# In the first MLP ScalarE casts the up weights' high parts, and the third token pair's first sums stand amid the second pair's chain

## The chip, the cores and the metric

The kernel runs on one core of a Trainium2 chip. The metric is the device time of one execution in microseconds; the median of three runs is given. Engines: TensorE (PE, matmuls; PEld, its weight loads), VectorE (DVE), ScalarE (ACT), GpSimd (POOL) and SyncE (SP, which issues most transfers). Each engine runs its own program in order; semaphores join them.

## What is computed

Clustered attention, then two MLPs, on 2 x 768 tokens of width 512, all in float32:

```python
h = x @ w_in                              # first MLP, d_ff 2048
g = h * (1.0 / (1.0 + np.exp(-1.702 * h)))
x = g @ w_out
...
h = x @ w_in                              # second MLP, d_ff 1024
e = np.exp(h - np.max(h, axis=-1, keepdims=True))
solu = h * (e / (np.sum(e, axis=-1, keepdims=True) + 1e-09))
mu = np.mean(solu, axis=-1, keepdims=True)
var = np.mean((solu - mu) ** 2, axis=-1, keepdims=True)
out = ((solu - mu) / np.sqrt(var + 1e-06) * g_ln) @ w_out
```

The attention (16 heads, keys of a query's own cluster only) is not touched by the change, except that its last turn also prepares the first weights of the first MLP.

## The kernel before

Each operand of a matmul is split in a high part (a cast to fp32r) and a low part (the exact value less the high one); a product is three matmuls: high x high, low x high, high x low. The cast and the subtraction are instructions of their own.

**First MLP.** There are three blocks (`bl`) of 512 tokens. A unit is one hidden tile of 128 columns; each block has 16, in pairs `m` (or `at`) with `u` = 0 and 1, so 48 units in all (n = 2 `at` + `u`). TensorE does, in turn, `up` of one unit (12 matmuls, L578 to L580) and `down` of the unit two before (12 matmuls, L593 to L595). For each unit:
- SP loads 512 KB of up and down weights into one of four slots of `gelu_raw`, as soon as `downl` of the unit four before is done (L453).
- GpSimd, `split_up`: a tiny `wait_scrap` instruction (L1354) that carries the waits, the cast `uph` (L1401), the difference `upl` (L1403). Then `split_down` of the unit before: `wait_scrap`, `downh` (L1411), `downl` (L1413). `uph[u]` may be written when `up` of the unit two before is done, `downh[u]` when its `down` is.
- ScalarE, `gelu`: the Tanh into `gate` (L786), then, when VectorE has multiplied the gate (L1028), the cast `gh` (L790). VectorE then makes `gl` (L1031).

`gate` is one buffer; `uph`, `upl`, `gh` and `gl` have two each. Beside this VectorE and ScalarE prepare the second MLP's weights: VectorE in the first block (`split_down_rows`), both in the second (`rhs_high` on ScalarE, `rhs_low_part` and `rhs_sum` on VectorE). At the end of a block ScalarE copies the four accumulators (`x2_high`, L796). ScalarE's and GpSimd's programs for this stage are partly loops.

**Second MLP.** There are six pairs of token tiles (`it` 0 to 5, tiles `u` 0 and 1). The up projection of a pair is a Strassen-like scheme of 7 products, in the order ONE, SIX, FIVE, SEVEN, TWO, FOUR, THREE (L685 to L687), which share few PSUM banks: TWO of a pair waits until ScalarE has copied ONE (`one_copy`, L897), FOUR until VectorE has used SIX (`u2_sum`, L1221), THREE until it has used SEVEN (`u3_sum`, L1233; between them `u4_sum`, L1228). Then come `c11`, `c21`, `c22`, `c12` (L1237 to L1251), and for each tile: max (L1260), exp (ACT, L904), solu and its mean (L1266 to L1274), the sum of squares (ACT, L919), variance (L1288, L1291), the root (POOL, L1508), the norm (L1296 to L1300, whose last instruction goes over the whole tile), transposes (PE, L705), `lnt_high` (ACT, L912) and `lnt_low` (DVE, L1280), and the down projection (L716 to L718), which `copy_out` (L927, L929) stores. GpSimd splits the next pair's left operands (L1495 to L1504), in its order before the two roots of the pair. TensorE does the transposes and the down projections of the pair before behind a pair's products. The order on each engine is written out by hand.

Of the kernel before, what the change touches and what calls it, by code (L numbers as in the profile page):

```python
# [16 lines left out]
def clustered_attention_two_mlps(nc, q_t, k_t, v_r, cent, w_gelu, w_ln, gains, out):  # L17
# [11 lines left out]
    DM = H * D  # L29
# [20 lines left out]
    with ExitStack() as ctx:  # L50
# [174 lines left out]
        uph_done = sem("uph_done")  # L225
# [27 lines left out]
        stat_step = sem("stat_step")  # L253
# [213 lines left out]
        def _(pe):  # L467
# [101 lines left out]
            def up(bl, m, u):  # L569
                n = bl * FF + m * 2 + u  # L570
                pe.wait_ge(uph_done, n + 1)
                pe.wait_ge(upl_done, n + 1)

                pe.wait_ge(gate_done[u], FREE + bl * (FF // 2) + m)
                tok = bass.ds(bl * BL, BL)
                for k in range(KT):
                    cols = slice(k * P, (k + 1) * P)
                    nc.tensor.matmul(hidden[u], uph[u][:, cols], xh[:, k, tok], start=k == 0, stop=False)  # L578
                    nc.tensor.matmul(hidden[u], uph[u][:, cols], xl[:, k, tok], start=False, stop=False)  # L579
                    last = nc.tensor.matmul(hidden[u], upl[u][:, cols], xh[:, k, tok], start=False, stop=k == KT - 1)  # L580
                last.then_inc(up_done[u], 1)
# [160 lines left out]
        def _(act):  # L742
# [38 lines left out]

            def gelu(at, u):
# [3 lines left out]
                nc.scalar.activation(gate[:], hidden[u], ACT.Tanh, scale=SLOPE / 2).then_inc(tanh_done, 1)  # L786
                act.wait_ge(gate_done[u], FREE + at + 1)
# [73 lines left out]
            with act.Fori(1, PER) as m:  # L861
                for u in range(2):
                    gelu(m, u)
            x2_high(0)
            for u in range(2):
                gelu(PER, u)
            act.wait_ge(ln_loaded, ITS * 16)
            for m in range(1, PER + 1):
                if m == PER:
                    x2_high(1)  # L870
                for u in range(2):
                    gelu(PER + m, u)
                    k, part = divmod((m - 1) * 2 + u, RHS_SLOTS)
                    if k < HK and part == 0:
                        rhs_high(B11, k, raw_unit(k, 0))
                    if k < HK and part == 1:
                        rhs_high(B21, k, raw_unit(HK + k, 0))
                    if k < HK and part == 2:
                        rhs_high(B22, k, raw_unit(HK + k, 1))
                    if k < HK and part == 4:  # L880
# [3 lines left out]
                    if k < HK and part == 5:  # L884
# [3 lines left out]
            with act.Fori(1, PER) as m:  # L888
                for u in range(2):
                    gelu((NBL - 1) * PER + m, u)  # L890
# [48 lines left out]
            for it in range(1, PAIRS):  # L939
                if it > 1:  # L940
                    one_copy(it)
                    lnt_high(it - 1, 0)
                for u in range(2):
                    exp_tile(it, u)
                    square(it, u)
                if it > 1:
                    copy_out(it - 2, 1)
                    lnt_high(it - 1, 1)
                copy_out(it - 1, 0)
                if it == 1:  # L950
                    lnt_high(0, 1)
# [8 lines left out]
        def _(dve):  # L960
# [241 lines left out]
            def solu_step(it, u):  # L1202
                return it * 8 + u * 3 + 2

            def variance_step(it, u):
                if it in (0, PAIRS - 1) and u == 1:
                    return it * 8 + 7
                return it * 8 + (6 if u else 3)

            def norm_step(it, u):  # L1210
                if it in (0, PAIRS - 1) and u == 0:
                    return it * 8 + 6
                return it * 8 + 6 + u + 1

# [48 lines left out]
            def solu_tile(it, u):  # L1263
# [8 lines left out]
                nc.vector.tensor_scalar(st(u, 5), st(u, 1), 1e-9, None, ALU.add).then_inc(stat_step, 1)  # L1272
                dve.wait_ge(stat_step, solu_step(it, u) - 1)
                nc.vector.reciprocal(st(u, 6), st(u, 5)).then_inc(stat_step, 1)  # L1274
# [9 lines left out]
            def variance(it, u):  # L1284
                dve.wait_ge(square_done, it * 2 + u + 1)
                dve.wait_ge(stat_step, solu_step(it, u))

                nc.vector.tensor_scalar(st(u, 7), st(u, 4), st(u, 6), st(u, 6), ALU.mult, ALU.mult  # L1288
                                        ).then_inc(stat_step, 1)
                dve.wait_ge(stat_step, variance_step(it, u))  # L1290
                nc.vector.tensor_scalar(st(u, 8), st(u, 7), 1.0 / F2, 1e-6, ALU.mult, ALU.add).then_inc(var_done, 1)  # L1291

            def norm_tile(it, u):
                t = it * 2 + u
                dve.wait_ge(root_done, t + 1)
                nc.vector.reciprocal(st(u, 10), st(u, 9)).then_inc(stat_step, 1)  # L1296
                dve.wait_ge(stat_step, norm_step(it, u))
# [37 lines left out]
        def _(pool):  # L1335
# [228 lines left out]
```

## Time and profile before

| | us |
|---|---|
| median of 3 runs | 671.42 (671.18 to 672.23) |
| the profiled execution | 671.9 |
| its span, first to last instruction | 670.1 |
| TensorE matmuls busy | 634.8 (95%) |
| weight loads busy | 532.0 (79%) |
| GpSimd busy | 492.6 (74%) |
| VectorE busy | 471.5 (70%) |
| ScalarE busy | 331.8 (50%) |
| first MLP | about 260 to 540 |
| second MLP | from about 525 on |

Records of matmuls overlap, since they are pipelined: in the first MLP one takes 0.39 us and the next starts 0.23 later, so a busy share near 100% says little there. The weight loads, one for each matmul, show TensorE's pace. The granted clock was 1.00 of full speed from 100 us on.

### The profile page before, as it was taken

What the parts mean: (1) busy time and instruction counts of PE and PEld (TensorE: products, weight loads), DVE (VectorE), ACT (ScalarE), POOL (GpSimd) and SP (SyncE); (2) the same over time, 40 slices, a digit from 0 to 9 for tenths busy, and PEclk for the clock granted to TensorE, in tenths of its full rate; (3) what the DMA queues carried; (4) which work ended last, traced back from release to release, by engine and by line L of the source; (5) the groups of instructions that cost most, each with busy time, mean ns of one, the idle gap of its engine ahead of it and who ended that gap; (6) DMA issues with size and microseconds to landing.
All of it is one profiled execution on the core that took longest, in us unless ns stands there. A gap on an engine that the chain in (4) does not pass through costs nothing.

```text
span 670.1 us, 11363 instructions
## 1 busy us (share of the span) xinstructions
PE 634.8 (95%) x3245; PEld 532.0 (79%) x3245; DVE 471.5 (70%) x805; ACT 331.8 (50%) x661; POOL 492.6 (74%) x680
## 2 busy tenths in 40 slices
PE   5679999999999999999999999999999997999998
PEld 1369989898989888788878778788888886888876
DVE  3769999999999985666646655734555587777660
ACT  1269999989999984222223322332222244443241
POOL 2667798797887977888878898988888778477100
PEclk9779999999999999999999999999999999999999
DMA  8866544545545421122232222222220000000001
GB/s 283 254 182 145 149 132 109 146 107 141 133 109 149 113 110 63 65 98 96 105 109 68 97 86 94 94 94 95 94 94 31 1 0 17 32 17 17 31 33 47
DMA packets 26937, 64.31 MB, mean 96 GB/s; under 512 B 3873, under 2 KB 10017, under 8 KB 26913
## 3 DMA queue, kind: packets, MB, share of 16 engines
q1 hardware_dynamic: 24896, 60.09, 30.1%
q10 hardware_dynamic: 2016, 3.93, 1.6%
q8 instruction: 11, 0.18, 0.1%
q14 instruction: 14, 0.11, 0.0%
HBM read 46.60 MB, written 4.72 MB: 77 GB/s over the span
## 4 chain that ended last, share of the span: by engine, by line
PE 66%; ACT 11%; DVE 8%; issue 8%; DMA 3%; POOL 3%; DVEq 1%; ACTq 0%; SPq 0%; POOLq 0%
PE banks L563 7%; PE banks L578 6%; PE banks L580 6%; PE banks L593 6%; PE banks L579 6%; PE banks L595 6%; PE banks L594 6%; PE banks L548 4%; ACT probs L805 4%; ACT probs_th L816 3%; PE banks L718 3%; PE banks L717 3%; PE banks L716 3%; PE banks L685 2%; PE banks L687 2%
## 5 line engine op out<-in xcount | busy, mean ns | idle before, releaser
L1057 DVE TENSOR_TENSOR probs_tl<-banks,probs_th 128x384 fp32r<-128x384 f32 x192 | 100.5, 546 | 11.3 <-ACT probs_th L816 8.8
L1037 DVE TENSOR_REDUCE neg_max<-banks 128x1 f32<-128x768 f32 x96 | 91.0, 949 | 10.2 <-PE banks L535 8.3
L816 ACT CAST probs_th<-banks 128x384 fp32r<-128x384 f32 x192 | 83.1, 486 | 23.3 <-PE banks L548 22.1
L1354 POOL TENSOR_TENSOR wait_scrap<-half_power 128x1 f32<-128x1 f32 x176 | 47.6, 270 | 63.8 <-DVE row_inv L1051 31.6
L1031 DVE TENSOR_TENSOR gl<-gate,gh 128x512 fp32r<-128x512 f32 x48 | 41.8, 871 | 71.4 <-ACT gh L790 71.4
L805 ACT ACTIVATE probs<-banks,neg_max 128x768 f32<-128x768 f32 x96 | 88.1, 918 | 6.1 <-DVE neg_max L1037 6.1
L1430 POOL TENSOR_SCALAR probs<-probs,row_inv 128x768 f32<-128x768 f32 x96 | 87.1, 908 | 0.0
L548 PE MATMUL banks<-ident,probs 128*128 128x128 f32 x576 | 79.4, 274 | 0.6 <-ACT hot_t L759 0.6
L563 PE MATMUL banks<-probs_th,v_parts 128*128 128x384 f32 x192 | 70.5, 367 | 9.9 <-DVE x_sums L1064 9.9
L790 ACT CAST gh<-gate 128x512 fp32r<-128x512 f32 x48 | 29.8, 621 | 100.9 <-PE banks L595 62.6
L578 PE MATMUL banks<-xh,uph 128*128 (+1 forms) x192 | 76.6, 399 | 1.2 <-POOL upl L1403 1.2
L1413 POOL TENSOR_TENSOR downl<-gelu_raw,downh 128x512 fp32r<-128x512 f32 x48 | 74.2, 1547 | 4.0
L593 PE MATMUL banks<-gh,downh 128*128 128x512 f32 x192 | 76.0, 396 | 0.2
L580 PE MATMUL banks<-xh,upl 128*128 (+1 forms) x192 | 75.5, 393 | 0.0
L595 PE MATMUL banks<-gh,downl 128*128 128x512 f32 x192 | 75.4, 393 | 0.0
L579 PE MATMUL banks<-xl,uph 128*128 (+1 forms) x192 | 75.1, 391 | 0.0
L594 PE MATMUL banks<-gl,downh 128*128 128x512 f32 x192 | 75.0, 391 | 0.0
L548 PEld LDWEIGHTS banks<-ident,probs 128*128 128x128 f32 x576 | 69.2, 141 | 4.7 <-ACT hot_t L759 0.9
L1403 POOL TENSOR_TENSOR upl<-gelu_raw,uph 128x512 fp32r<-128x512 f32 x48 | 63.9, 1332 | 4.0
L786 ACT ACTIVATE gate<-banks 128x512 f32<-128x512 f32 x48 | 28.7, 598 | 76.6 <-PE banks L580 63.4
L563 PE MATMUL banks<-probs_tl,v_parts 128*128 128x384 f32 x192 | 65.3, 340 | 0.0
L531 PE MATMUL banks<-k_high,q_parts 128*128 128x384 f32 x192 | 56.5, 376 | 5.0 <-DMA k_low<-mask_rows 2.3
(144 smaller groups left out, 1415.0 us busy)
## 6 DMA issues: line engine op xcount, KB each, us to landing
gelu_raw<-w_gelu SPq DMA_DIRECT2D x48, 512.0 KB, 3.3
ln_raw<-w_ln SPq DMA_DIRECT2D x8, 512.0 KB, 4.5
pair_t<-q_t SPq DMA_DIRECT2D x4, 768.0 KB, 7.4
pair_t<-k_t SPq DMA_DIRECT2D x4, 768.0 KB, 8.2
kq_raw<-k_t SPq DMA_DIRECT2D x16, 192.0 KB, 3.5
kq_raw<-q_t SPq DMA_DIRECT2D x16, 192.0 KB, 3.7
q_parts<-k_high SPq DMA_DIRECT2D x16, 192.0 KB, 2.6
q_high<-k_high SPq DMA_DIRECT2D x16, 192.0 KB, 3.0
```

The costliest lines, as they stand in the source:

```text
L548: last = nc.tensor.transpose(pt_bank(n, c)[:, t * P:(t + 1) * P], probs[:, n % NP, k * P:(k + 1) * P], ident[:])
L563: last = nc.tensor.matmul(head_out, v_parts[j][:, i // 2].rearrange("p two d -> p (two d)"), part[half % 2][:, i // 2, :], start=i == 0, s ...
L578: nc.tensor.matmul(hidden[u], uph[u][:, cols], xh[:, k, tok], start=k == 0, stop=False)
L579: nc.tensor.matmul(hidden[u], uph[u][:, cols], xl[:, k, tok], start=False, stop=False)
L580: last = nc.tensor.matmul(hidden[u], upl[u][:, cols], xh[:, k, tok], start=False, stop=k == KT - 1)
L593: nc.tensor.matmul(acc[d], downh[u][:, cols], gh[u][:], start=first, stop=False)
L594: nc.tensor.matmul(acc[d], downh[u][:, cols], gl[u][:], start=False, stop=False)
L595: last = nc.tensor.matmul(acc[d], downl[u][:, cols], gh[u][:], start=False, stop=end)
L805: nc.scalar.activation(probs[:, n % NP, :].rearrange("p (c t) -> p c t", c=2), scores[n % 2], ACT.Exp, bias=neg_max[:, n % NP:n % NP + 1], ...
L816: nc.scalar.copy(probs_th[half % 2][:, c * CH:(c + 1) * CH, i * P:(i + 1) * P], pt_bank(n, c).rearrange("p (t s) -> p t s", t=CH)).then_in ...
L1037: nc.vector.tensor_reduce(out=neg_max[:, col], in_=scores[n % 2], op=ALU.max, axis=mybir.AxisListType.XY, negate=True).then_inc(max_done, 1)
L1057: nc.vector.tensor_tensor(probs_tl[half % 2][at], pt_bank(n, c).rearrange("p (t s) -> p t s", t=CH), probs_th[half % 2][at].bitcast(F32), ...
```

## The change

1. For units 4 to 47 the cast `uph` moves from GpSimd to ScalarE (`up_high`), directly behind the Tanh of the unit two before, with the wait for the load. GpSimd keeps the four casts of units 0 to 3, without their `wait_scrap`. `uph_done` becomes two semaphores.
2. ScalarE's loops over the first MLP are written out.
3. In the second MLP pair 2's `one_copy`, `u2_sum`, `u4_sum` and `u3_sum` are done amid pair 1's exp and solu, as is `lnt_high(0, 1)` and `lnt_low(0, 1)`; `norm_tile(1, 0)` comes behind `u3_sum(2)`.
4. The counting semaphore `stat_step` becomes four, one for each kind of small step.

```diff
             def up(bl, m, u):
                 n = bl * FF + m * 2 + u
-                pe.wait_ge(uph_done, n + 1)
+                pe.wait_ge(uph_done[u], bl * (FF // 2) + m + 1)
                 pe.wait_ge(upl_done, n + 1)
...
+            def up_high(at, u):
+                n = at * 2 + u
+                act.wait_ge(gelu_loaded[n % RAW], (n // RAW + 1) * 16)
+                nc.scalar.copy(uph[u][:], gelu_raw[:, n % RAW, 0:DM]).then_inc(uph_done[u], 1)
+
             def gelu(at, u):
                 act.wait_ge(up_done[u], at + 1)
 
                 act.wait_ge(gl_done, FREE + at * 2 + u)
                 nc.scalar.activation(gate[:], hidden[u], ACT.Tanh, scale=SLOPE / 2).then_inc(tanh_done, 1)
+                if at >= 1 and (at + 1) * 2 + u < NBL * FF:
+                    up_high(at + 1, u)
                 act.wait_ge(gate_done[u], FREE + at + 1)
...
             for it in range(1, PAIRS):
-                if it > 1:
-                    one_copy(it)
+                if it == 1:
+                    exp_tile(1, 0)
+                    lnt_high(0, 1)
+                    square(1, 0)
+                    one_copy(2)
+                    exp_tile(1, 1)
+                    square(1, 1)
+                    copy_out(0, 0)
+                else:
+                    if it > 2:
+                        one_copy(it)
                     lnt_high(it - 1, 0)
...
             for it in range(PAIRS):
-                u2_sum(it)
-                if it >= 2:
+                if it != 2:
+                    u2_sum(it)
+                if it >= 3:
                     norm_tile(it - 1, 0)
-                u4_sum(it)
-                u3_sum(it)
+                if it != 2:
+                    u4_sum(it)
+                    u3_sum(it)
                 if it == 1:
                     lnt_low(0, 0)
+                if it == 2:
+                    norm_tile(1, 0)
                 if it >= 1:
                     norm_tile(it - 1, 1)
...
                 variance(it, 0)
+                if it == 1:
+                    lnt_low(0, 1)
+                    u2_sum(2)
+                    u4_sum(2)
                 solu_tile(it, 1)
+                if it == 1:
+                    u3_sum(2)
                 if it in (0, PAIRS - 1):
                     norm_tile(it, 0)
                 variance(it, 1)
-                if it >= 1:
+                if it > 1:
                     lnt_low(it - 1, 1)
...
             def split_up(it, r):
                 u = r % 2
-                pool.wait_ge(gelu_loaded[r], (it + 1) * 16)
-                if exists(it, r, 2, RAW):
-
-                    pool.wait_ge(up_done[u], it * (RAW // 2) + r // 2)
-                carry_waits(STEPS + r)
                 raw = gelu_raw[:, r, 0:DM]
-                nc.gpsimd.tensor_scalar(uph[u][:], raw, 1.0, 1.0, ALU.mult, ALU.mult).then_inc(uph_done, 1)
-                pool.wait_ge(uph_done, it * RAW + r + 1)
+                if isinstance(it, int):
+                    pool.wait_ge(gelu_loaded[r], 16)
+                    if r >= 2:
+
+                        pool.wait_ge(up_done[u], r // 2)
+                    nc.gpsimd.tensor_scalar(uph[u][:], raw, 1.0, 1.0, ALU.mult, ALU.mult).then_inc(uph_done[u], 1)
+                pool.wait_ge(uph_done[u], it * 2 + r // 2 + 1)
                 nc.gpsimd.tensor_tensor(upl[u][:], raw, uph[u][:].bitcast(F32), ALU.subtract).then_inc(upl_done, 1)
```

GpSimd's loop over the first MLP, one unit, before (L1402, L1408 and L1412 only set up registers and waits):

```order
L1354 TENSOR_TENSOR wait_scrap<-half_power 128x1
L1401 TENSOR_SCALAR uph<-gelu_raw 128x512
L1402 ISA
L1403 TENSOR_TENSOR upl<-gelu_raw,uph 128x512
L1408 ISA
L1354 TENSOR_TENSOR wait_scrap<-half_power 128x1
L1411 TENSOR_SCALAR downh<-gelu_raw 128x512
L1412 ISA
L1413 TENSOR_TENSOR downl<-gelu_raw,downh 128x512
```

and now:

```order
L1408 TENSOR_TENSOR upl<-gelu_raw,uph 128x512
L1413 ISA
L1359 TENSOR_TENSOR wait_scrap<-half_power 128x1
L1416 TENSOR_SCALAR downh<-gelu_raw 128x512
L1417 ISA
L1418 TENSOR_TENSOR downl<-gelu_raw,downh 128x512
```

The first `wait_scrap` and the cast have left GpSimd's program; the rest keeps its order. On ScalarE the cast stands between the Tanh and `gh`, here at the start of the second block, now:

```order
L806 ACTIVATE x_sums<-banks 128x512 x4
L794 ACTIVATE gate<-banks 128x512
L788 CAST uph<-gelu_raw 128x512
L800 CAST gh<-gate 128x512
L794 ACTIVATE gate<-banks 128x512
L788 CAST uph<-gelu_raw 128x512
L800 CAST gh<-gate 128x512
```

VectorE from the max of tile (1,1) to the norm of (1,0), before (L1266 to L1274 solu, L1288 and L1291 variance, L1280 `lnt_low(0, 1)`, L1221, L1228 and L1233 the sums of pair 2, L1296 to L1300 the norm):

```order
L1260 TENSOR_REDUCE stat<-gelu_raw 128x1
L1288 TENSOR_SCALAR stat<-stat 128x1
L1291 TENSOR_SCALAR stat<-stat 128x1
L1266 ISA gelu_raw,stat<-gelu_raw,exp 128x1024
...
L1288 TENSOR_SCALAR stat<-stat 128x1
L1291 TENSOR_SCALAR stat<-stat 128x1
L1280 TENSOR_TENSOR xh<-banks,xh 128x1024
L1221 TENSOR_TENSOR hid<-banks,hid 128x512
L1296 RECIPROCAL stat<-stat 128x1
L1298 TENSOR_TENSOR stat<-stat 128x1
L1300 TENSOR_SCALAR gelu_raw<-gelu_raw,stat 128x1024
L1228 TENSOR_TENSOR hid<-banks,hid 128x512
L1233 TENSOR_TENSOR hid<-banks,hid 128x512
```

and now (L1275 `lnt_low`, L1216, L1223 and L1228 the sums, L1261 to L1269 solu, L1283 and L1286 variance, L1291 to L1295 the norm):

```order
L1255 TENSOR_REDUCE stat<-gelu_raw 128x1
L1283 TENSOR_SCALAR stat<-stat 128x1
L1286 TENSOR_SCALAR stat<-stat 128x1
L1275 TENSOR_TENSOR xh<-banks,xh 128x1024
L1216 TENSOR_TENSOR hid<-banks,hid 128x512
L1223 TENSOR_TENSOR hid<-banks,hid 128x512
L1261 ISA gelu_raw,stat<-gelu_raw,exp 128x1024
...
L1228 TENSOR_TENSOR hid<-banks,hid 128x512
L1283 TENSOR_SCALAR stat<-stat 128x1
L1286 TENSOR_SCALAR stat<-stat 128x1
L1291 RECIPROCAL stat<-stat 128x1
L1293 TENSOR_TENSOR stat<-stat 128x1
```

The low parts and two sums have moved ahead of the solu of (1,1), the third sum behind it. ScalarE at the same place, before (L904 exp, L919 square, L927 and L929 `copy_out(0, 0)`, L912 `lnt_high(0, 1)`, L897 `one_copy(2)`):

```order
L904 ACTIVATE exp,stat<-gelu_raw,stat 128x1024
L919 ACTIVATE gelu_raw,stat<-gelu_raw,stat 128x1024
L904 ACTIVATE exp,stat<-gelu_raw,stat 128x1024
L919 ACTIVATE gelu_raw,stat<-gelu_raw,stat 128x1024
L927 COPY gelu_raw<-banks 128x512
L929 DMA out<-gelu_raw 128x512
L912 CAST xh<-banks 128x1024
L897 COPY hid<-banks 128x512
```

and now:

```order
L906 ACTIVATE exp,stat<-gelu_raw,stat 128x1024
L914 CAST xh<-banks 128x1024
L921 ACTIVATE gelu_raw,stat<-gelu_raw,stat 128x1024
L899 COPY hid<-banks 128x512
L906 ACTIVATE exp,stat<-gelu_raw,stat 128x1024
L921 ACTIVATE gelu_raw,stat<-gelu_raw,stat 128x1024
L929 COPY gelu_raw<-banks 128x512
L931 DMA out<-gelu_raw 128x512
```

The two copies that stood last come in between the exp and the squares.

## Rows read from the trace of the kernel before

**Rows 1.** Stretches: us, busy time (x instructions) of PE, PEld, DVE, ACT, POOL, clock, DMA

```profile
275.41:330.49 55.08, 55.07 (x240) 45.02 (x240) 36.67 (x36) 12.19 (x20) 46.29 (x60) 1.00 0.28 95
353.15:435.78 82.63, 81.75 (x349) 64.79 (x349) 52.10 (x55) 25.58 (x44) 73.62 (x88) 1.00 0.26 89
443.91:510.30 66.39, 66.39 (x289) 54.16 (x288) 35.41 (x42) 15.23 (x25) 55.28 (x72) 1.00 0.26 87
```

**Rows 2.** Waits of PEld, 340 to 446 us: total us, times, longest

```profile
PEld banks L578 <- issue: 3.6, 8, 0.7
PEld banks L593 <- DVE gl L1031: 0.5, 1, 0.5
```

**Rows 3.** Timeline, first block's start: start us, us, engine, what [idle before]

```profile
272.77 0.38 POOL L1354 TENSOR_TENSOR wait_scrap<-half_power 128x1 f32<-128x1 f32 x1
...
275.41 0.19 PEld L578 LDWEIGHTS banks<-xh,uph 128*128 128x128 f32 x1 [0.87 <-issue]
```

**Rows 4.** Timeline of PEld, pair 2 of the second MLP

```profile
561.32 0.19 PEld L685 LDWEIGHTS banks<-rhs_h,lhs_h 128*128 128x128 f32 x1 [2.60 <-POOL lhs_l L1497]
561.42 0.19 PEld L686 LDWEIGHTS banks<-rhs_l,lhs_h 128*128 128x128 f32 x1
...
565.78 0.19 PEld L685 LDWEIGHTS banks<-rhs_h,lhs_h 128*128 128x128 f32 x1 [1.85 <-POOL lhs_l L1497]
...
567.04 1.03 PEld L705 LDWEIGHTS banks<-ident,gelu_raw 128*128 128x128 f32 x8
```

**Rows 5.** Timeline of ACT, pairs 1 and 2

```profile
557.56 1.15 ACT L919 ACTIVATE gelu_raw<-gelu_raw,stat 128x1024 f32<-128x1024 f32 x1 [1.49 <-DVE stat L1270]
...
559.70 1.01 ACT L912 CAST xh<-banks 128x1024 fp32r<-128x1024 f32 x1 [0.43 <-ACT gelu_raw L927]
560.61 0.59 ACT L897 COPY hid<-banks 128x512 f32<-128x512 f32 x1
```

**Rows 6.** Timeline of DVE, pairs 1 and 2

```profile
556.11 1.23 DVE L1266 CUSTOM_DVE_ANT_0 gelu_raw<-gelu_raw,exp 128x1024 f32<-128x1024 f32 x1 [0.93 <-ACT exp L904]
...
560.75 1.22 DVE L1280 TENSOR_TENSOR xh<-banks,xh 128x1024 fp32r<-128x1024 f32 x1 [1.45 <-ACT xh L912]
...
564.97 0.69 DVE L1233 TENSOR_TENSOR hid<-banks,hid 128x512 f32<-128x512 f32 x1
```

**Rows 7.** POOL's groups by form, 300 to 500 us: busy us, mean ns | idle

```profile
L1401 POOL TENSOR_SCALAR uph<-gelu_raw 128x512 fp32r<-128x512 f32 x36 | 25.3, 704 | 0.0
L1354 POOL TENSOR_TENSOR wait_scrap<-half_power 128x1 f32<-128x1 f32 x72 | 25.1, 348 | 23.5 <-PE banks L595 20.4 <-PE banks L580 2.9
```

**Rows 8.** ACT's groups by form, 300 to 500 us

```profile
L859 ACT CAST rhs_h<-ln_raw 128x512 fp32r<-128x512 f32 x14 | 8.2, 616 | 0.0
```

**Rows 9.** Timeline, start of the third block

```profile
441.58 0.60 ACT L786 ACTIVATE gate<-banks 128x512 f32<-128x512 f32 x1 [0.64 <-PE banks L580]
...
442.21 0.69 DVE L1028 SCALAR_TENSOR_TENSOR gate<-gate,banks 128x512 f32<-128x512 f32 x1 [5.52 <-ACT gate L786]
...
442.55 1.29 POOL L1403 TENSOR_TENSOR upl<-gelu_raw,uph 128x512 fp32r<-128x512 f32 x1
...
443.91 0.19 PEld L578 LDWEIGHTS banks<-xh,uph 128*128 128x128 f32 x1
```

**Rows 10.** Timeline, one unit of the second block

```profile
387.78 1.66 POOL L1413 TENSOR_TENSOR downl<-gelu_raw,downh 128x512 fp32r<-128x512 f32 x1
...
395.74 0.60 ACT L786 ACTIVATE gate<-banks 128x512 f32<-128x512 f32 x1 [2.13 <-PE banks L580]
```

**Rows 11.** The page's DMA issues: KB each, median us to landing

```profile
gelu_raw<-w_gelu SPq DMA_DIRECT2D x48, 512.0 KB, 3.3
```

**Rows 12.** Timeline of PE, transposes of tile (0,1)

```profile
552.60 1.03 PE L705 MATMUL banks<-ident,hid 128*128 128x128 f32 x8
```

**Rows 13.** Tile `gelu_raw`: ns min/median/max, first and last start

```profile
L1300 DVE TENSOR_SCALAR gelu_raw<-gelu_raw,stat x6: 810/814/1315, 563.0 to 648.4; 128x1024 f32<-128x1024 f32 x6
```

**Rows 14.** Timeline of DVE, low part of tile (1,0)

```profile
571.20 1.22 DVE L1280 TENSOR_TENSOR xh<-banks,xh 128x1024 fp32r<-128x1024 f32 x1
```

More of the change, by code:

```diff
@@ L224, in clustered_attention_two_mlps @@
         gelu_loaded = [sem(f"gelu_loaded{r}") for r in range(RAW)]
-        uph_done = sem("uph_done")
+        uph_done = two_sems("uph_done")
         upl_done = sem("upl_done")
@@ L252, in clustered_attention_two_mlps @@
         square_done = sem("square_done")
-        stat_step = sem("stat_step")
+        sum2_guarded = sem("sum2_guarded")
+        sum2_inverted = sem("sum2_inverted")
+        spread_scaled = sem("spread_scaled")
+        root_inverted = sem("root_inverted")
         var_done = sem("var_done")
@@ L859, in rhs_high @@
                 nc.scalar.copy(rhs_h[:, i, k, :], src).then_inc(rhs_high_done, 1)
-            with act.Fori(1, PER) as m:
-                for u in range(2):
[L863 to L874, printed above, removed]
+            for at in range(1, NBL * PER):
+                if at == PER + 1:
+                    act.wait_ge(ln_loaded, ITS * 16)
+                if at % PER == 0:
+                    x2_high(at // PER - 1)
+                for u in range(2):
+                    gelu(at, u)
+                    k, part = divmod((at - PER - 1) * 2 + u, RHS_SLOTS)
+                    if 0 <= k < HK and part == 0:
                         rhs_high(B11, k, raw_unit(k, 0))
-                    if k < HK and part == 1:
+                    if 0 <= k < HK and part == 1:
                         rhs_high(B21, k, raw_unit(HK + k, 0))
-                    if k < HK and part == 2:
+                    if 0 <= k < HK and part == 2:
                         rhs_high(B22, k, raw_unit(HK + k, 1))
-                    if k < HK and part == 4:
+                    if 0 <= k < HK and part == 4:
                         act.wait_ge(rhs_summed, k * 4 + 2)
@@ L883, in _ @@
                         rhs_high(T3, k, raw_unit(k, 1))
-                    if k < HK and part == 5:
+                    if 0 <= k < HK and part == 5:
                         act.wait_ge(rhs_summed, k * 4 + 4)
@@ L887, in _ @@
                         rhs_high(T4, k, raw_unit(HK + k, 0))
-            with act.Fori(1, PER) as m:
-                for u in range(2):
-                    gelu((NBL - 1) * PER + m, u)
             def one_copy(it):
@@ L939, in _ @@
             for it in range(1, PAIRS):
-                if it > 1:
-                    one_copy(it)
+                if it == 1:
[9 more added lines that the diff above has]
+                        one_copy(it)
                     lnt_high(it - 1, 0)
[L943 to L946, printed above, removed]
+                    for u in range(2):
+                        exp_tile(it, u)
+                        square(it, u)
                     copy_out(it - 2, 1)
                     lnt_high(it - 1, 1)
-                copy_out(it - 1, 0)
-                if it == 1:
-                    lnt_high(0, 1)
+                    copy_out(it - 1, 0)
             lnt_high(PAIRS - 1, 0)
@@ L1199, in st @@
                 return stat[:, u, i:i + 1]
[L1202 to L1213, printed above, removed]
             def quarter(it, u, c):
@@ L1270, in solu_tile @@
                 nc.vector.tensor_scalar(st(u, 3), st(u, 2), -1.0 / F2, None, ALU.mult).then_inc(mean_done, 1)
-                nc.vector.tensor_scalar(st(u, 5), st(u, 1), 1e-9, None, ALU.add).then_inc(stat_step, 1)
-                dve.wait_ge(stat_step, solu_step(it, u) - 1)
-                nc.vector.reciprocal(st(u, 6), st(u, 5)).then_inc(stat_step, 1)
+                nc.vector.tensor_scalar(st(u, 5), st(u, 1), 1e-9, None, ALU.add).then_inc(sum2_guarded, 1)
+                dve.wait_ge(sum2_guarded, t + 1)
+                nc.vector.reciprocal(st(u, 6), st(u, 5)).then_inc(sum2_inverted, 1)
             def lnt_low(it, u):
@@ L1295, in norm_tile @@
                 dve.wait_ge(root_done, t + 1)
-                nc.vector.reciprocal(st(u, 10), st(u, 9)).then_inc(stat_step, 1)
-                dve.wait_ge(stat_step, norm_step(it, u))
+                nc.vector.reciprocal(st(u, 10), st(u, 9)).then_inc(root_inverted, 1)
+                dve.wait_ge(root_inverted, t + 1)
                 nc.vector.tensor_tensor(st(u, 11), st(u, 10), st(u, 6), ALU.mult).then_inc(scale_done, 1)
```

6 lines of the change are left out of this document (3 added, 3 removed).

## The prediction

> **What bounds the kernel now.** I read the stretches first, then the waits of TensorE's weight loads, then the chain around the stalls. In the first MLP TensorE is nearly always busy, so what counts is how far it is from its own pace. One weight load belongs to each matmul, so the loads are a clock. The last block's stretch is the undisturbed pace: 66.39 us for 288 loads, 0.2305 us each, 5.53 us for the 24 matmuls of one hidden tile of 128 (a unit) [rows 1]. (The count in each row includes the load that starts at the window's end.) The second block's stretch took 82.63 us for 348 loads; at the last block's pace it would take 80.2, so it **lost 2.4 us**. The first block's stretch, 55.08 for 240 loads, lost nothing (55.3 at that pace). The list of waits says where: before the up matmuls (L578) 8 waits, 3.6 us, between 340 and 446 us, with "issue" as the cause, and one of 0.5 before L593 that is put down to VectorE's `gl` [rows 2]. "Issue" isn't a proof of GpSimd, but what an up matmul waits for is `upl`, GpSimd's last product of a unit.
>
> At the start of the first block the same wait is larger: the load at 275.41 came after 0.87 us of idling, right behind the `wait_scrap` of 0.38 us that began on GpSimd at 272.77, the cast and `upl` [rows 3].
>
> In the second MLP TensorE stands still twice, in the third token pair (pair 2): 2.60 us before the load at 561.32 and 1.85 before that at 565.78 [rows 4]. The engine named there (GpSimd) is a false lead: the first wait ends with ScalarE's copy `hid` (L897), which starts at 560.61 and takes 0.59 [rows 5]; the second with VectorE's third sum (L1233), 564.97 plus 0.69 [rows 6]. A wait shows 0.04 us more than it costs, since undisturbed loads lie 0.23 apart and last 0.19; and the load after a wait follows after 0.10 instead of 0.23. So the two cost 2.60 + 1.85 - 2 x 0.17 = **4.1 us**.
>
> **The change part by part: first MLP.** For 44 of 48 units GpSimd loses the cast `uph`, 704 ns in the mean between 300 and 500 us, and one `wait_scrap` of 348 ns [rows 7]: 1.05 us of the unit's 5.53. GpSimd's order is downl of one unit, then upl of the next, and the down part waits for TensorE to free `downh`; that loop is what came out longer than TensorE's pace when VectorE's extra work in the second block slowed GpSimd. With 1.05 us less in it, each of the eight waits (3.6/8, below 0.5 on average) goes. Value: 2.4 us. The wait at 275.41 goes too: `uph` for this unit can be cast after the Tanh of unit 2, before GpSimd is free at 272.77, and 1.0 us, the scrap's 0.38 [rows 3] and a cast of some 0.62 [rows 8], disappears. Value: 0.83 (its 0.87 less 0.04); but the first block then runs at 0.2305 a load, not 55.08/240, which gives back 0.24. From below the value of these three is nothing (if GpSimd isn't the cause), from above 3.3 with the smaller irregularities between the blocks.
>
> What ScalarE gets is 44 casts. The row for such a cast is 616 ns (`rhs_h`, same shape) [rows 8]. It stands between the Tanh (0.60) and `gh`, while VectorE multiplies the gate: undisturbed, `gh` starts some 1.35 us after the Tanh's start, after a Tanh of 0.60 and a gate of 0.69 [rows 9], and Tanh plus cast is over after 1.2. So it is hidden by VectorE's work. If that cover were gone, it would cost `gh` 0.6 us, which has to be ready for a down product over one unit later, so still nothing.
>
> Two places have no slack: the first units of blocks two and three. Their `uph` waits for the up product before last and is wanted one product later. Before, GpSimd began on it 0.1 us after the Tanh's start. Now it is Tanh, cast, `upl`: 441.58 + 0.55 + 0.62 + 0.05 + 1.29 = 444.1, and TensorE, which loaded at 443.91 [rows 9], loads at 444.2. I put +0.3 on this place, +0.1 on the one before (a wait there already), and the 0.5 before L593 stays, since VectorE's order is the same. First MLP: 2.4 + 0.8 - 0.24 - 0.4 = **2.5 us gained**.
>
> The cast also waits for its weights. The load into a slot goes out when `downl` of four units earlier ends (387.78 + 1.66 = 389.44) and lands after 3.3 us in the median, about 392.9; the Tanh behind which the cast stands is at 395.74 [rows 10, 11]. 3 us of slack: nothing. Queued behind a late one would be `gh`, then `gl`, then the down product.
>
> **Second MLP.** I follow the new order with the old durations. The transposes of tile (0,1) end at 553.63 [rows 12]. ScalarE copies them (L912) from 553.67, next instruction 0.91 later, as from 559.70 to 560.61 [rows 5]: the square of (1,0) starts at 554.58 and is done 1.25 later (1.15 [rows 5] and 0.1 for reading out its sum), 555.83; the copy of product ONE is done at 556.3 instead of 561.2; exp of (1,1) at 557.5. VectorE: variance to 556.3, `lnt_low` 1.2 [rows 6] to 557.5, first sum (0.69 as the third [rows 6], and the handover) to 558.2, second to 558.95, then solu of (1,1), whose mean is there 1.4 us later (1.23 and the small operations), 560.4, third sum to 561.3. The square of (1,1) lies beside it, 560.4 to 561.7; variance to 562.15; norm of (1,0): 0.4 of small operations and a tile that takes between 0.81 and 1.31 [rows 13]; I take 1.31, since GpSimd takes up its splits at just that time: 563.9.
> TensorE goes from 558.76 (561.32 less the wait) through TWO and FOUR without a wait, is at THREE at 561.5 (third sum 561.3) and at the transposes of (1,0) at 562.9. They wait for the norm: load at 564.0 instead of 567.04 [rows 4], 3.0 earlier. So **a new wait of 1.1 us** stands there. Next late is `lnt_low` of (1,0): VectorE finishes the norm of (1,1) at 565.5, needs 4.0 from c11 to `lnt_low` (now from 567.2, when the norm after the third sum is done, to 571.20) and 1.22 for it [rows 14]: 570.7, while TensorE comes at 564.0 + 6.5 = 570.5 (eight transposes, 1.0, and 24 matmuls, 5.53). 0.3 lost. In pair 3 the copies and sums still end over 1 us ahead of TensorE. GpSimd's splits for pair 3 start 2.8 us later (behind the root of (1,1)) and were ready some 7 us early. Second MLP: 3.0 - 0.3 and 0.1 for the quicker load after a wait: **2.8 us gained**; bounds 1.2 and 4.1.
>
> Sum: 5.3 us. The profiled execution took 671.9 us (span 670.1), the median of three is 671.42, so 671.9 - 5.3 = 666.6 for such a run and **666.1** for the median.
>
> What the norm tile takes may be settled by a rule. The Trainium skill, SBUF — State Buffer, "Who interferes with whom": a VectorE operation in a two-port mode and GpSimd take turns on a shared port pair, and whichever starts first keeps it for the whole instruction. By that rule the tile (0.81 or 1.31 in the rows) would start behind the root at 562.75 and run at 0.81, the sum would be 0.3 larger, and the time 665.8; the trace has both durations, but no row that says why.
>
> **The rivals.**
> 1. Forecast, 62%: 665.0 to 667.2.
> 2. Everything goes, 12%: no new wait at the transposes and none at the block starts. 3.3 + 4.1 = 7.4: 664.0. For it: norm at 0.81. Against: the chain exp, solu, square, variance, norm is serial.
> 3. VectorE is slower amid the interleaved sums, 13%: each of some six operations between 556 and 564 meets GpSimd and takes 0.3 longer; the transposes wait till 565.6, second MLP 1.2: 667.7.
> 4. The "issue" waits aren't GpSimd's, 6%: they stay, and the first MLP gives only the start less the block starts, about 0.2: 668.4. Then the change doesn't do what it says there.
> 5. Slower, 4%: the weights land late and the cast holds `gh`. The slack is 3 us, and `gh` has a further 1.6 before its old start; from about 8 us landing time on, against 3.3 measured, TensorE waits in each unit. 0.2 us in 44 units is 8.8, less 5.3: 674.9. Against it: no row of the stage comes near.
> The rest, 3%, is no change.
>
> **How the numbers follow.** Cases 1 to 4 lie between 664.0 and 668.4, so the range is 664.1 to 668.3; ends are the two bounds of the unknown costs. What can be told from no change is about 0.2% (1.3 us). Faster: cases 1 to 4, 93%; same 3%; slower 4%.
>
> **What would show it.** Right: no wait over 0.3 us before L578's successor from 355 to 435 us, `upl` ready a microsecond or more before its matmul; ScalarE's cast directly behind each Tanh with `gh` still 1.36 after it; 1.1 us of waiting before the transposes of (1,0), none before TWO, and about 2.7 less at the next transposes. Wrong: ScalarE waits for a DMA in front of the cast; the second block still takes over 82 us; VectorE's sums of pair 2 well after 561.3.

## The result and the profile after

The changed kernel took 666.82 us (median of 6, 664.11 to 669.46) against 671.75 (median of 6) for the kernel before: a ratio of 0.9925, 95% interval 0.9899 to 0.9951, or 4.9 us less. The forecast was 666.1, 5.3 less. Two single executions of the experiments below (714.20 us in e1, 2606.30 us in e8) were far slower and are left out of the ratios.

The profiled execution of the changed kernel took 669.46 us (span 667.6), the longest of its six. Comparing spans would say 2.5 us. So I cut both executions at the first up product of the first MLP and at the first `down` of the last two units, from where all work depends on the MLPs alone. Stretches of the kernel before (columns as in [rows 1]):

```profile
251.65:530.89 279.24, 277.79 (x1214) 225.13 (x1214) 160.55 (x177) 75.67 (x131) 232.68 (x296) 1.00 0.24 83
530.89:670.10 139.21, 132.09 (x620) 107.79 (x618) 91.90 (x181) 52.73 (x81) 66.45 (x94) 1.00 0.06 23
```

and of the changed one:

```profile
255.21:532.12 276.91, 276.52 (x1214) 225.37 (x1213) 161.13 (x177) 98.07 (x175) 191.95 (x206) 1.00 0.24 84
532.12:667.60 135.48, 131.86 (x620) 107.62 (x618) 91.67 (x181) 52.54 (x81) 65.68 (x94) 1.00 0.07 24
```

From the first up product on the gain is 2.33 + 3.73 = **6.1 us** (2.5 + 2.8 were forecast). What is missing in that one execution lies ahead of it: the first up product came at 255.21 and not 251.65. Of these 3.6 us, 3.2 are there at the first weight load of `k_high` (34.29 against 31.12), before which TensorE waits for loads that both kernels issue alike; in the changed kernel's profile:

```profile
30.22 0.20 PEld L485 LDWEIGHTS banks<-pair_t,c_diag 128*32 128x32 f32 x8 [4.74 <-DMA pair_t<-k_t]
```

Whether the change has a part in that is asked of the experiments. The casts: ScalarE is busy 98 us instead of 76 in the first MLP, GpSimd 192 instead of 233.

The stretches of the three blocks, which answer to [rows 1]:

```profile
278.16:333.49 55.33, 55.33 (x241) 45.05 (x240) 31.70 (x37) 17.28 (x30) 37.97 (x40) 1.00 0.28 99
356.26:436.89 80.63, 80.41 (x349) 65.25 (x349) 56.51 (x55) 33.21 (x59) 58.79 (x60) 1.00 0.26 91
445.25:511.53 66.28, 66.28 (x288) 53.98 (x288) 38.09 (x42) 21.83 (x38) 44.96 (x48) 1.00 0.25 87
```

The first is 0.25 longer, as worked out (0.24): it runs at 0.2305 a load. The second is 2.0 shorter, the third 0.1. The waits of weight loads, 340 to 450 us, answer to [rows 2]; L581 is the old L578, L596 the old L593:

```profile
PEld banks L596 <- issue: 1.2, 2, 0.6
PEld banks L581 <- issue: 0.6, 2, 0.3
```

Eight waits, 3.6 us in all, before the up products have become two, 0.6 in all, and both are the first units of blocks two and three. But before the downs it is two, 1.2 in all. One of them closely:

```profile
345.75 0.69 DVE L1039 TENSOR_TENSOR gl<-gate,gh 128x512 fp32r<-128x512 f32 x1 [0.70 <-ACT gh L800]
345.90 1.69 POOL L1418 TENSOR_TENSOR downl<-gelu_raw,downh 128x512 fp32r<-128x512 f32 x1
```

```profile
347.82 0.19 PEld L596 LDWEIGHTS banks<-gh,downh 128*128 128x128 f32 x1 [0.58 <-issue]
```

`downl` of the block's last unit ends at 347.59 and the load follows 0.23 later. At a block's end TensorE does three downs in a row, so between the one that frees a `downh` and the one that needs it again there is a single down, 2.8 us, and no up product. GpSimd's scrap, cast and subtraction took 2.56 here, from 345.03 on, and the load was due at 347.28. In the kernel before the same load (344.69) waited 0.5 for VectorE's `gl` [rows 2], while `downl` had ended at 344.09, 0.1 before the load was due:

```profile
342.80 1.29 POOL L1413 TENSOR_TENSOR downl<-gelu_raw,downh 128x512 fp32r<-128x512 f32 x1
```

```profile
343.09 1.55 DVE L1031 TENSOR_TENSOR gl<-gate,gh 128x512 fp32r<-128x512 f32 x1 [0.69 <-ACT gh L790]
```

There GpSimd began first and VectorE took 1.55; in the changed kernel VectorE began first (345.75) and took 0.69, and GpSimd took 1.69. So the wait changed sides with the order in which the two began; that the one caused the other isn't shown by a run.

GpSimd's and ScalarE's groups by form, 300 to 500 us, against [rows 7, 8]:

```profile
L1408 POOL TENSOR_TENSOR upl<-gelu_raw,uph 128x512 fp32r<-128x512 f32 x36 | 54.3, 1509 | 6.9 <-ACT uph L788 6.9
...
L1359 POOL TENSOR_TENSOR wait_scrap<-half_power 128x1 f32<-128x1 f32 x36 | 8.4, 234 | 51.2 <-PE banks L598 51.2
```

```profile
L788 ACT CAST uph<-gelu_raw 128x512 fp32r<-128x512 f32 x36 | 22.0, 612 | 0.0
```

The cast costs 612 ns (616 forecast). GpSimd now waits 51 us for TensorE (`downh` free again) where it waited 20, and 7 for ScalarE's cast, so inside a block it isn't the bound any more. The 0.0 of idling before ScalarE's casts says that the weights were always there.

One unit of the second block shows the order (410 to 418 us): Tanh, the cast directly behind it, and `upl` of the next up product already under way:

```profile
414.37 1.74 POOL L1408 TENSOR_TENSOR upl<-gelu_raw,uph 128x512 fp32r<-128x512 f32 x1
...
414.62 0.60 ACT L794 ACTIVATE gate<-banks 128x512 f32<-128x512 f32 x1 [1.57 <-PE banks L583]
...
415.11 0.61 ACT L788 CAST uph<-gelu_raw 128x512 fp32r<-128x512 f32 x1
...
416.97 0.19 PEld L581 LDWEIGHTS banks<-xh,uph 128*128 128x128 f32 x1
...
417.44 0.62 ACT L800 CAST gh<-gate 128x512 fp32r<-128x512 f32 x1 [1.72 <-PE banks L598]
```

That `upl` ends at 416.11, 0.86 before its load at 416.97; in the kernel before the distance was 0.34 or less for all but one unit of this block. (Over the block it is now 0.74 to 1.30; the prediction's sign was a microsecond or more.) `gh` waits 1.7 us more for TensorE: the cast lies beside a wait. Where nothing held `gh` up, at 362.97 behind a Tanh at 361.62, it still came 1.35 behind it, as forecast (1.36).

In the second MLP the times of the changed kernel lie 1.23 later than in the kernel before (transposes of tile (0,0) at 543.00 and 541.77). The weight loads of pair 2, against [rows 4]; L708 are the transposes:

```profile
564.35 0.86 PEld L708 LDWEIGHTS banks<-ident,gelu_raw 128*128 128x128 f32 x8 [0.32 <-DVE gelu_raw L1295]
...
571.17 0.86 PEld L708 LDWEIGHTS banks<-ident,gelu_raw 128*128 128x128 f32 x8 [0.57 <-issue]
```

The waits before TWO and THREE are gone. The transposes of (1,0) wait 0.3 for the norm, those of (1,1) 0.57 for `lnt_low(1, 0)`. ScalarE and VectorE there, against [rows 5, 6]:

```profile
554.90 1.02 ACT L914 CAST xh<-banks 128x1024 fp32r<-128x1024 f32 x1 [1.71 <-PE banks L708]
555.82 1.15 ACT L921 ACTIVATE gelu_raw<-gelu_raw,stat 128x1024 f32<-128x1024 f32 x1
...
556.96 0.57 ACT L899 COPY hid<-banks 128x512 f32<-128x512 f32 x1
```

```profile
559.98 1.22 DVE L1261 CUSTOM_DVE_ANT_0 gelu_raw<-gelu_raw,exp 128x1024 f32<-128x1024 f32 x1
...
561.57 0.69 DVE L1228 TENSOR_TENSOR hid<-banks,hid 128x512 f32<-128x512 f32 x1
...
563.48 0.81 DVE L1295 TENSOR_SCALAR gelu_raw<-gelu_raw,stat 128x1024 f32<-128x1024 f32 x1
...
569.84 1.21 DVE L1275 TENSOR_TENSOR xh<-banks,xh 128x1024 fp32r<-128x1024 f32 x1
```

Less 1.23, the copy ends at 556.3 (forecast 556.3), the third sum at 561.0 (561.3), the norm's tile runs 562.25 to 563.06 (forecast to 563.9) and `lnt_low` ends at 569.8 (570.7).

### The profile page after: what moved, and what is told of

It reads as the page before. It is cut to its first block, busy times and chain, and to the rows that moved or that the text cites. A ratio compares the mean times of both kernels' runs of the same rounds, so it can differ in the third digit from the quotient of the medians.

```text
span 667.6 us, 11191 instructions
## 1 busy us (share of the span) xinstructions
PE 630.4 (94%) x3245; PEld 529.9 (79%) x3245; DVE 471.6 (71%) x805; ACT 354.4 (53%) x705; POOL 451.9 (68%) x588
## 4 chain that ended last, share of the span: by engine, by line
PE 67%; ACT 10%; issue 7%; DVE 6%; DMA 4%; POOL 4%; DVEq 1%; SPq 1%; ACTq 0%; POOLq 0%
PE banks L581 7%; PE banks L583 7%; PE banks L582 7%; PE banks L596 6%; PE banks L566 6%; PE banks L598 6%; PE banks L597 6%; ACT probs L815 4%; PE banks L551 4%; ACT probs_th L826 3%; PE banks L721 2%; PE banks L720 2%; PE banks L719 2%; ACT x_sums L832 2%; PE banks L690 2%
## 5 line engine op out<-in xcount | busy, mean ns | idle before, releaser
L1359 POOL TENSOR_TENSOR wait_scrap<-half_power 128x1 f32<-128x1 f32 x128 | 26.6, 208 | 97.7 <-PE banks L598 66.9
L1039 DVE TENSOR_TENSOR gl<-gate,gh 128x512 fp32r<-128x512 f32 x48 | 40.3, 840 | 63.4 <-ACT gh L800 63.4
L1418 POOL TENSOR_TENSOR downl<-gelu_raw,downh 128x512 fp32r<-128x512 f32 x48 | 75.9, 1582 | 4.0
L596 PE MATMUL banks<-gh,downh 128*128 128x512 f32 x192 | 76.1, 396 | 0.4 <-POOL downl L1418 0.2
L581 PE MATMUL banks<-xh,uph 128*128 (+1 forms) x192 | 76.0, 396 | 0.0
L1408 POOL TENSOR_TENSOR upl<-gelu_raw,uph 128x512 fp32r<-128x512 f32 x48 | 71.0, 1479 | 7.2 <-ACT uph L788 6.9
L1036 DVE SCALAR_TENSOR_TENSOR gate<-gate,banks 128x512 f32<-128x512 f32 x48 | 32.7, 682 | 42.8 <-ACT gate L794 42.8
```

The source lines that it names most:

```text
L596: nc.tensor.matmul(acc[d], downh[u][:, cols], gh[u][:], start=first, stop=False)
```

## The experiments

Differences of the stages are taken from each kernel's profile between the same loads of TensorE; in the changed kernel's two executions they repeat within 0.05 us, apart from the start. "To the end" is from the first up product on: 418.4 us before, 412.4 in the changed kernel. Timed medians stand beside their own runs of the kernel before.

**One part at a time.** e1_first_mlp_only takes the first MLP's edits alone, e2_second_mlp_only the second MLP's. The edit of e1 against the changed kernel, and that of e2:

```diff
 # e1: ScalarE and VectorE in the second MLP as before
-                if it == 1:
-                    exp_tile(1, 0)
-                    lnt_high(0, 1)
...
 # e2: GpSimd casts all of uph, ScalarE's loops as before
-                if at >= 1 and (at + 1) * 2 + u < NBL * FF:
-                    up_high(at + 1, u)
```

> Only the first MLP's part of the change (the casts on ScalarE, its loops written out); the second MLP as before. Theory A (the two parts gain apart and add up, as the two profiles say when aligned at the first up product: 2.3 us of 6.1): about 2.3 us under the kernel before, and in the second MLP the waits of 2.6 and 1.9 us before TWO and THREE of pair 2 are back. Rival B (the written-out program of ScalarE costs time in the first 60 us, where the profiled execution of the changed kernel was 3.6 us late): the gain is 1 us or less, and the first up product of this kernel starts near 255 us and not near 252.

Measured: 670.71 against 672.56, ratio 0.9968 (0.9954 to 0.9982). Its stages:

```profile
251.58:528.41 276.83, 276.45 (x1214) 225.35 (x1214) 161.19 (x177) 98.06 (x175) 192.07 (x206) 1.00 0.25 84
528.41:667.60 139.19, 132.12 (x620) 107.58 (x618) 91.66 (x181) 52.75 (x81) 66.61 (x94) 1.00 0.06 23
```

> Only the second MLP's part (the order of ScalarE and VectorE in pairs 1 and 2, four semaphores for one); the first MLP as before. Theory A: 3.7 us under the kernel before, with a wait of about 0.3 before the transposes of tile (1,0) and 0.6 before those of (1,1). Rival B: the full gain of the changed kernel, 4.9, since ScalarE's program in the first MLP is the short one.

Measured: 667.49 against 672.56, ratio 0.9922 (0.9904 to 0.9940). Its stages:

```profile
251.31:530.47 279.16, 277.64 (x1214) 224.74 (x1214) 160.57 (x177) 75.71 (x131) 232.67 (x296) 1.00 0.25 83
530.47:665.90 135.43, 131.83 (x620) 107.61 (x618) 91.65 (x181) 52.52 (x81) 65.62 (x94) 1.00 0.07 24
```

e1 gains 2.4 us in the one stage and nothing in the other, e2 0.1 and 3.8. The parts are independent and add up to 6.3, within 0.2 of the changed kernel's 6.1. The timed gains (1.9 and 5.1 us) add up to 7, where the whole change was timed at 4.9 and, a second time (below), at 6.0: that is how far such medians carry here.

**Is it GpSimd's time?** e3_gpsimd_busy_again gives GpSimd scrap and cast back, with a result that nobody reads; `uph` comes from ScalarE:

```diff
                 pool.wait_ge(uph_done[u], it * 2 + r // 2 + 1)
+                if not isinstance(it, int):
+                    carry_waits(STEPS + r)
+                    nc.gpsimd.tensor_scalar(exp2[:, 0:DM].bitcast(F32R), raw, 1.0, 1.0, ALU.mult, ALU.mult)
                 nc.gpsimd.tensor_tensor(upl[u][:], raw, uph[u][:].bitcast(F32), ALU.subtract).then_inc(upl_done, 1)
```

> The changed kernel, with GpSimd doing for units 4 to 47 a wait_scrap and a cast of the same size again, whose result nobody reads (it goes into exp2); uph still comes from ScalarE. Theory A (what GpSimd no longer does in each unit is the gain of the first MLP): the small waits before the up products of the second block return, its stretch of 348 loads takes 82 to 83 us and not 80.6, the start of the first block loses 0.8, and the time is 2 to 2.8 us above the changed kernel. Rival (the gain comes from the cast being early, whoever does it): as the changed kernel, within 0.5 us.

Measured: 669.66 against 672.56, ratio 0.9954; to the end 415.7. The first MLP takes 3.3 us more than in the changed kernel (2 to 2.8 were expected) and 1.0 more than in the kernel before; the second block's stretch and its waits:

```profile
355.22:437.39 82.17, 81.58 (x348) 64.86 (x348) 52.23 (x55) 33.22 (x59) 74.09 (x88) 1.00 0.27 89
```

```profile
PEld banks L581 <- issue: 3.7, 5, 1.1
PEld banks L581 <- POOL upl L1411: 0.9, 2, 0.5
```

1.5 of the 2.0 us gained in that stretch are lost again, 0.6 of the 0.8 at the start, and the two block starts cost 0.7 each on top, as GpSimd's work there begins only when ScalarE's cast is over. So GpSimd's 1.05 us a unit are the cause of most of the gain. The 0.5 and 0.2 us that didn't come back may be what the early cast is worth; no run separates that.

e9_scrap_back gives back the scrap alone (the middle line of that edit):

> The changed kernel with only the wait_scrap back on GpSimd before upl, 0.35 us of the 1.05 a unit that it lost. In the changed kernel upl is ready 0.85 to 1.3 us before its matmul. Theory: as long as what is added is less than that, nothing: the second block's stretch stays at 80.6 to 80.8 us (with scrap and cast back it was 82.2). Rival (each piece of GpSimd's time counts in proportion): a third of the loss, 81.2 us.

Measured in one run, 666.71: to the end 412.6, the second block's stretch 80.5:

```profile
353.54:434.08 80.54, 80.44 (x348) 65.29 (x348) 52.93 (x55) 33.19 (x59) 63.79 (x74) 1.00 0.27 91
```

GpSimd is busy 5 us more in it and TensorE isn't slower. Only the first block's end and the two block starts lose 0.14 each, and the second block's end gains 0.13. So inside a block GpSimd's time has a point below which it costs nothing, and this lies between 0.35 and 1.05 us a unit above that of the changed kernel.

**Is the cast covered?** e4_cast_twice doubles it:

```diff
+                nc.scalar.copy(exp2[:, 0:DM].bitcast(F32R), gelu_raw[:, n % RAW, 0:DM])
                 nc.scalar.copy(uph[u][:], gelu_raw[:, n % RAW, 0:DM]).then_inc(uph_done[u], 1)
```

> The changed kernel with ScalarE's cast done twice for each of units 4 to 47, first into a part of exp2 that nobody reads, then into uph: what the cast costs if it isn't covered. The prediction's theory (ScalarE has room between the Tanh and gh, and gh isn't due for over a unit): nothing in the blocks themselves, stretches of 55.3, 80.6 and 66.3 us as in the changed kernel; only the first unit of blocks two and three, where the cast is waited for, loses some 0.5 us each. Rival (ScalarE's in-order time counts, each gh is pushed back and TensorE with it): some 0.3 to 0.6 us in each of 44 units, over 13 us in all.

Measured in one run, 665.70: to the end 413.2, 0.9 more; the first two stretches:

```profile
273.49:328.82 55.33, 55.33 (x242) 45.05 (x240) 33.00 (x38) 22.47 (x40) 38.28 (x40) 1.00 0.30 96
352.09:432.70 80.61, 80.40 (x348) 65.25 (x349) 57.26 (x55) 40.91 (x74) 58.34 (x60) 1.00 0.28 91
```

Unchanged to 0.02 us, and 0.50 and 0.51 more at the two block starts. A second cast costs nothing 42 times of 44 and its length twice: the cast itself is covered except at these two places.

**Does the written-out program cost anything?** e8_loops_kept runs blocks one and three of ScalarE's `gelu` in loops of two pairs:

```diff
-            for at in range(1, NBL * PER):
...
+                with act.Fori(first, last) as j:
+                    for d in range(2):
+                        for u in range(2):
+                            gelu(j * 2 + d, u, ((d * 2 + 2 + u) % RAW, j + d))
```

> The changed kernel with ScalarE's loops kept: blocks one and three of the first MLP run as a loop over two pairs of units, the casts included; the same work in the same order. Theory A (a longer program costs nothing): as the changed kernel, within 0.5 us. Rival B (writing the loops out costs about 1 us at the start, in fetching the program or in the order in which the first loads land): 1 us faster than the changed kernel, with the first up product near 252 us.

Measured: 667.23 against 672.56, ratio 0.9913 (0.9892 to 0.9934); to the end 412.3, the first up product at 252.9. That is the changed kernel's time, and not 1 us less. And e10_changed_again, the changed kernel timed a second time:

> The changed kernel as it is, timed again beside the version above. Theory (the stages repeat to 0.1 us, and only the time until attention runs evenly varies): from the first up product to the end 412.4 us again, 6.1 under the kernel before, whatever the whole time is; the median 5 to 6 us under the kernel before. Rival (the change costs about 1 us at the start): the first up product again 1 us or more later than in the kernel before, in the median gain 5 or less.

Measured: 666.88 against 672.85, 6.0 less, ratio 0.9917 (0.9899 to 0.9936); to the end 412.3, the first up product at 251.6:

```profile
251.58:528.44 276.86, 276.48 (x1214) 225.53 (x1214) 161.18 (x177) 98.02 (x175) 191.83 (x206) 1.00 0.25 84
528.44:663.90 135.46, 131.83 (x620) 107.72 (x618) 91.67 (x181) 52.52 (x81) 65.56 (x94) 1.00 0.07 24
```

The first up product stands at 251.65 in the kernel before, at 255.2 and 251.6 in two executions of the changed one, and between 250.7 and 253.5 in the eight other kernels of this study, whose attention is the same. Of those eight, the six with ScalarE's loops all written out start at 250.7 to 253.5, the two that keep loops (e2, e8) at 251.3 and 252.9. So the 3.6 us at the start don't come with the change; a cost of the long program there isn't seen. One below 1 us can't be excluded by so few starts.

**Which of the two stalls counted?** e12_copy_only leaves VectorE's order of the second MLP as before and keeps ScalarE's new one, so that the copy of ONE is early and the sums are late:

```diff
-                if it != 2:
-                    u2_sum(it)
+                u2_sum(it)
...
-                if it == 1:
-                    lnt_low(0, 1)
-                    u2_sum(2)
-                    u4_sum(2)
```

> The changed kernel with VectorE's order of the second MLP as before; ScalarE's new order (lnt_high and the copy of product ONE amid pair 1) stays. Theory: the larger wait, 2.6 us before TWO of pair 2, had ScalarE's copy as its last releaser, but the third sum at VectorE sets the end: TWO runs at once, TensorE then waits longer before FOUR and THREE, and from the transposes of (0,0) to those of (1,0) it is 25.3 us as in the kernel before (21.3 in the changed one). Rival (the waits add up, each worth what it shows): 2.4 us of the 4.0 are gained, 22.9 us.

Measured in one run, 673.38 against one of 673.12: 26.0 us from the transposes of (0,0) to those of (1,0), where the kernel before has 25.3, and 7.8 instead of 6.5 to those of (1,1). The wait before TWO moved to FOUR; the two waits are 4.15 us together and were 4.45:

```profile
561.90 0.19 PEld L688 LDWEIGHTS banks<-rhs_h,lhs_h 128*128 128x128 f32 x1 [2.44 <-POOL lhs_l L1492]
...
562.93 0.19 PEld L690 LDWEIGHTS banks<-rhs_h,lhs_l 128*128 128x128 f32 x1
564.83 0.29 PEld L688 LDWEIGHTS banks<-rhs_h,lhs_h 128*128 128x128 f32 x1 [1.71 <-POOL lhs_sums L1499]
...
565.42 0.33 PEld L690 LDWEIGHTS banks<-rhs_h,lhs_l 128*128 128x128 f32 x1
565.85 0.33 PEld L688 LDWEIGHTS banks<-rhs_h,lhs_h 128*128 128x128 f32 x1
```

THREE begins 23.7 us behind the transposes of (0,0), where it was 24.0: the order of ScalarE alone gains 0.3 us of the 3.9. From there to the end it took 2.4 us more than the kernel before, since the clock had fallen (last section). The reverse, VectorE's order alone, wasn't run, nor were its moved instructions (`lnt_low`, the sums, the norm) tried one by one.

**A version meant to be better.** e7_four_edits (three edits, the first at two places):

```diff
+                ahead = u == 0 and at in (FF // 2, FF)
+                if ahead:
+                    up_high(at + 1, u)
...
-                if it >= 3:
+                if it >= 4:
                     norm_tile(it - 1, 0)
...
-                if it == 2:
-                    norm_tile(1, 0)
+                if it in (2, 3):
+                    norm_tile(it - 1, 0)
...
                 c21_sum(it)
+                if it == 2:
+                    lnt_low(1, 0)
```

> A version meant to be better than the changed kernel; edits: (a) at the first unit of blocks two and three ScalarE casts before its Tanh and not behind it; (b) in pair 2 lnt_low of tile (1,0) comes before c22 and not behind c12; (c) in pair 3 the second and third sum come before the norm of (2,0). Theory: (a) takes 0.2 to 0.3 off each of the two block starts, (b) takes the 0.5 us of waiting before the transposes of (1,1), (c) the 0.1 before THREE of pair 3; in all 1.0 us under the changed kernel, which only the profile can show, as the start varies by more. Rival (b moves the wait): max, exp and solu of pair 2 come 1.1 us later, and a wait of 0.3 to 1 us appears in pair 3.

Measured: 666.50 against 672.85, ratio 0.9901 (0.9879 to 0.9922); to the end 411.7, 0.6 less than the changed kernel. 1.0 was expected. By stage: the block starts 0.28 and 0.21 less, the step to the transposes of (1,1) 0.53 less, all as expected; but the stretches behind these three places are 0.16, 0.11 and 0.16 longer, and the 0.1 expected in pair 3 didn't come. After a wait TensorE regains some of it, so a wait taken away is worth less than it shows. The rival's wait in pair 3 didn't come either. By their timed medians the two kernels can't be told apart; by the profile this one is the best.

## Why the prediction was right

The time (666.8 for 666.1) and the direction came out, mostly for the reasons given. That the time came so close owes something to luck: by stage the gain was 6.1 where 5.3 was forecast, and errors of both signs stand in it. Step by step, forecast and measured:

| step | forecast | measured |
|---|---|---|
| wait at the first block's start goes | -0.83 | -0.81 |
| first block back at TensorE's own pace | +0.24 | +0.25 |
| second block's stretch | -2.4 | -2.0 |
| start of block two | +0.1 | -0.02 |
| start of block three | +0.3 | +0.23 |
| second MLP up to the transposes of (1,0) | -3.0 | -3.92 |
| from there to the transposes of (1,1) | +0.3 | +0.34 |
| to the next transposes | -0.1 | -0.16 |
| sum; measured with +0.13 (first block's end) and -0.11 (third block) | -5.4 | -6.1 |

The prediction rounded 2.56 for the first MLP down to 2.5 and so came to 5.3.

- That GpSimd's time was the cause behind "issue" is shown by e3, for 1.5 of the 2.0 us, and by e9.
- The cover of the cast is shown by e4. The two places without slack, named ahead, are exactly those that lose 0.5 us when it is doubled.
- Mis-sized: **"each of the eight waits (3.6/8, below 0.5 on average) goes"**, 2.4 us. The up waits did, but the stretch of 2.4 held the wait at the block's end too, 0.5 before a down. It is there in the changed kernel too: `downl` between two downs ends 0.24 before the load in both (435.54 and 435.78 before), and the change doesn't touch it. At the first block's end I had expected the 0.5 to stay "since VectorE's order is the same"; it stayed with GpSimd as releaser, since `gl` took 0.69 and `downl` 1.69 where they had taken 1.55 and 1.29. A right number with a wrong reason.
- Mis-sized: **"a tile that takes between 0.81 and 1.31 [rows 13]; I take 1.31"**. It took 0.81, and it began 0.3 earlier than the chain of operations before it had been added up to. So the new wait was 0.3 and not 1.1, and the transposes came 0.9 earlier than forecast. The rule of the Trainium skill (SBUF — State Buffer, "Who interferes with whom") gave the right length, 0.81, but not by the way it was used: the tile was to start behind the root, and the trace has it start 0.23 behind the root's start. The trace agrees that one of the two runs at full speed and the other is held back: the root on GpSimd took 1.08 us instead of 0.55, until the norm's tile, begun at 563.48, was over at 564.29. It doesn't show the rule's order, that the first to start keeps the ports: the root had begun first and ended late all the same. (Only its end: the next instruction on GpSimd began 0.52 later, at 563.77, as behind the root at 559.38 before.) The next norm tile, begun at 564.76, 0.12 behind a subtraction on GpSimd that took its usual 0.74, took 1.17. Nothing here shows what decides between the lengths.

```profile
563.25 1.08 POOL L1513 TENSOR_TENSOR stat<-stat,half_power 128x1 f32<-128x1 f32 x1 [4.40 <-DVE stat L1286]
```

- Wrong, though small: **"in pair 3 the copies and sums still end over 1 us ahead"**. The third sum of pair 3 ended just in time, at 585.63, and a load came at 585.75 that was due at 585.67; the next one, at 585.90, was on time again, so it cost nothing. The norm of (2,0), ahead of it on VectorE, took 1.38; with 0.81 it would still have been only 0.6 ahead.
- The gain from the first up product on is 6.1 us, the timed one 4.9 at first and 6.0 when timed again (e10). The difference between the two timings is no larger than what the start varies by.

## What to carry to other kernels

When TensorE is near its own pace, measure that pace in an undisturbed stretch and count each stretch's loads against it: the difference is all there is to gain, and it showed where. A stall's releaser is only the last of those it waits for: making ScalarE's copy early alone (e12) gained 0.3 us of 3.9. And where executions differ by several microseconds before the part that was changed, compare stage by stage; there differences of 0.1 us repeat.

## What was not expected

- **The clock fell in e12, and the waits don't explain it.** From the load at 564.83 (rows above) to 569.7 the loads lie 0.43 us apart instead of 0.23. The column behind GpSimd's is the granted clock; 0.50 is 1.2 GHz of 2.4:

```profile
559.50:561.90 2.40, 0.38 (x2) 0.00 (x1) 2.24 (x6) 0.53 (x2) 1.66 (x3) 1.00 0.29 109
561.90:563.20 1.30, 1.27 (x6) 1.05 (x6) 1.26 (x2) 0.00 (x0) 1.04 (x2) 0.99 0.00 0
563.20:570.00 6.80, 5.69 (x18) 4.39 (x17) 6.25 (x11) 0.50 (x1) 5.85 (x9) 0.50 0.01 2
570.00:580.00 10.00, 10.00 (x48) 8.16 (x48) 6.46 (x16) 6.21 (x11) 5.47 (x9) 1.00 0.01 2
```

It fell at 563.2, while TensorE was at the six matmuls between its two waits, 1.3 us after the first wait (2.44) and before the second; the last of the six, begun at 563.15, took 0.60 instead of 0.39. In the kernel before TensorE had waited 2.60 and was then busy too, and the clock stayed at 1.00 throughout. So neither the second wait nor its nearness can be the cause; one execution shows the fall, and what makes the difference stays open. From THREE to the end it cost some 2.4 us.
- **TensorE regains part of a wait.** The load after the first one behind a wait follows after 0.10 to 0.11 instead of 0.23, and the stretch behind it is a little shorter: the first block's 240 loads took 55.08 us right behind a wait of 0.87 in the kernel before, and 55.33 without it.
- **The start varies by 3 us** between two executions of the changed kernel (first load of `k_high` at 34.29 and at 31.16), in waits for the first loads (4.7 us in one place of the first profile). That is more than most single edits here are worth.
